# At most one kq and one kvt load under way in the retention, and two w1 loads

## The reference

```python
# q, k, v: 4 batches x 8 heads x 576 tokens x 64
scores = q @ k.T / sqrt(64)
ret = scores * D            # D[i, j] = gamma_head ** (i - j) for i >= j, else 0
x = (ret @ v)               # -> 2304 tokens x 512
h = x @ w_in                # 512 x 2048
g = where(h >= 1, h, where(h <= -1, 0, (h + 1) ** 2 / 4))
x = g @ w_out               # 2048 x 512
out = ((x @ w_a) * (x @ w_b)) @ w_out2    # 512 x 1536, 1536 x 512
```

## Time and profile before

| | |
|---|---|
| runs | 885.16, 887.18, 887.47 us |
| profiled execution | 886.08 us, of which the span 884.1 us |
| PE / PEld / DVE / ACT / POOL busy | 866.7 / 774.3 / 481.0 / 334.8 / 36.7 us |
| granted TensorE clock | 1.00 over the span |
| DMA | 137.46 MB, mean 155 GB/s |
| loads of the retention, us from issue to landing (median) | kq 6.7, kvt 5.9, w1 8.4 |

### The profile page before, as it was taken

How to read it: one execution, slowest core, us unless ns; L and a number is a source line. 1 busy time by engine, 2 the same in 40 slices (tenths; PEclk the granted TensorE clock), 3 DMA queues, 4 the chain that set the end, 5 groups by cost and what they waited for, 6 DMA issues and landing times.

```text
span 884.1 us, 13516 instructions
## 1 busy us (share of the span) xinstructions
PE 866.7 (98%) x5488; PEld 774.3 (88%) x5488; DVE 481.0 (54%) x831; ACT 334.8 (38%) x598; POOL 36.7 (4%) x54
## 2 busy tenths in 40 slices
PE   6889999999999999999999999999999999999998
PEld 6887888888899888888889999999999999999996
DVE  4685665655566755565663633574434574434443
ACT  1235555444454644444442433342223242223220
POOL 4550000000000000000000000000000000000000
PEclk9999999999999999999999999999999999999999
DMA  9997000023233022222345644545454845454622
GB/s 355 313 339 297 0 1 1 22 111 113 113 151 136 8 110 112 114 114 108 138 167 179 251 166 162 197 152 203 153 204 165 275 168 214 167 215 167 222 64 71
DMA packets 33453, 137.46 MB, mean 155 GB/s; under 512 B 2672, under 2 KB 12912, under 8 KB 28784
## 3 DMA queue, kind: packets, MB, share of 16 engines
q1 hardware_dynamic: 33248, 136.27, 42.2%
q10 hardware_dynamic: 144, 0.33, 0.1%
HBM read 109.86 MB, written 26.74 MB: 154 GB/s over the span
## 4 chain that ended last, share of the span: by engine, by line
PE 97%; DMA 1%; issue 1%; SPq 0%; DVE 0%; ACT 0%; POOL 0%; DVEq 0%; ACTq 0%; POOLq 0%
PE score_b L541 6%; PE score_b L545 6%; PE score_b L543 6%; PE score_a L545 4%; PE score_a L543 4%; PE score_a L541 4%; PE score_a L495 4%; PE kv_b L512 4%; PE score_b L495 4%; PE ret_b L512 4%; PE score_a L497 4%; PE score_a L496 4%; PE kv_b L513 4%; PE kv_b L514 4%; PE score_b L496 4%; PE ret_b L513 4%
## 5 line engine op out<-in xcount | busy, mean ns | idle before, releaser
L739 DVE TENSOR_TENSOR gate_w<-relu_s,relu_r 128x512 f32<-128x512 f32 (+1 forms) x80 | 51.0, 638 | 99.1 <-ACT relu_r L917 99.0
L541 PE MATMUL score_b<-xop_hi,wop 128*128 128x384 f32 x288 | 96.8, 336 | 0.1
L545 PE MATMUL score_b<-xop_hi,wop 128*128 128x384 f32 x288 | 96.7, 336 | 0.0
L543 PE MATMUL score_b<-xop_lo,wop 128*128 128x384 f32 x288 | 96.5, 335 | 0.0
L926 ACT ACTIVATE gh<-gated 128x512 fp32r<-128x512 f32 (+1 forms) x80 | 47.2, 590 | 105.9 <-DVE gated L742 105.9
L748 DVE TENSOR_TENSOR gl<-gated,gh 128x512 fp32r<-128x512 f32 (+1 forms) x80 | 51.1, 639 | 50.8 <-ACT gh L926 50.6
L541 PE MATMUL score_a<-xop_hi,wop 128*128 128x384 f32 x216 | 72.2, 334 | 0.0
L545 PE MATMUL score_a<-xop_hi,wop 128*128 128x384 f32 x216 | 72.2, 334 | 0.0
L543 PE MATMUL score_a<-xop_lo,wop 128*128 128x384 f32 x216 | 72.2, 334 | 0.0
L976 ACT ACTIVATE p<-score_b 128x384 f32<-128x384 f32 x36 | 17.7, 491 | 105.3 <-PE score_b L545 105.3
L541 PEld LDWEIGHTS score_b<-xop_hi,wop 128*128 128x128 f32 x288 | 54.1, 188 | 2.0 <-ACT p L976 0.4
(11 more groups left out here) (131 smaller groups left out, 2141.6 us busy)
## 6 DMA issues: line engine op xcount, KB each, us to landing
wop<-w_ops SPq DMA_DIRECT2D x36, 1792.0 KB, 7.3
w_ops<-op_hi SPq DMA_DIRECT2D x12, 896.0 KB, 4.6
w_ops<-op_lo SPq DMA_DIRECT2D x12, 896.0 KB, 6.4
kq<-k_q SPq DMA_DIRECT2D x16, 576.0 KB, 6.7
wo_raw<-w_out SPq DMA_DIRECT2D x9, 1024.0 KB, 9.7
kvt<-kv_tok SPq DMA_DIRECT2D x16, 512.0 KB, 5.9
ab_raw<-w_ab SPq DMA_DIRECT2D x12, 512.0 KB, 3.6
w1a_raw<-w SPq DMA_DIRECT2D x10, 512.0 KB, 8.4
```

The costliest lines, as they stand in the source:

```text
L541: pe.matmul(o, w[:, 0, at], xop_hi[b][:, k, :], start=(start and k == 0), stop=False, skip_group_check=True)
L543: pe.matmul(o, w[:, 0, at], xop_lo[b][:, k, :], start=False, stop=False, skip_group_check=True)
L545: mm = pe.matmul(o, w[:, 1, at], xop_hi[b][:, k, :], start=False, stop=(k == 1), skip_group_check=True)
L739: nc.vector.tensor_tensor(gate_w[:, 0:WIDTHS[t]], relu_s[:, 0:WIDTHS[t]], relu_r[:, 0:WIDTHS[t]], ALU.add).then_inc(gatew_ready, 1)
```

## The change

Three waits are added, all on SP. Before `kq` of unit n it waits until `kq` of unit n-1 has landed, before `kvt` of unit n until `kvt` of unit n-1 has landed, and before `w1` block f until block f-2 has landed. Nothing else is altered.

```diff
                     sp.wait_ge(scores_ready, 2 * (n - SLOTS) + 2)
                     sp.wait_ge(q_ready, n - SLOTS + 1)
+
+                if n:
+                    sp.wait_ge(kq_loaded[(n - 1) % SLOTS], 16 * ((n - 1) // SLOTS + 1))
                 sp.dma_start(kq[:, s, :, :], k_q[n]).then_inc(kq_loaded[s], 16)
                 if n >= SLOTS:
                     sp.wait_ge(kv_ready, n - SLOTS + 1)
                     sp.wait_ge(inner_done, n - SLOTS + 1)
+                if n:
+                    sp.wait_ge(kvt_loaded[(n - 1) % SLOTS], 16 * ((n - 1) // SLOTS + 1))
                 sp.dma_start(kvt[:, s, :, :, :], kv_tok[n]).then_inc(kvt_loaded[s], 16)
                 sp.dma_start(vtail[0:TAIL, s, :], v_tail[n]).then_inc(vtail_loaded[s], 16)
 
             def load_w1(f):
+                if f >= 2:
+                    sp.wait_ge(w1_loaded[f - 2], 16)
                 sp.dma_start(w1_raw(f), w1[f]).then_inc(w1_loaded[f], 16)
```

## The result

The changed kernel takes 901.34 us (median of 4 runs, 898.70 to 903.25), the kernel before 887.06: the ratio is 1.0163, with a 95% interval of 1.0133 to 1.0193. It is slower, by 1.3 to 1.9%, and outside the range that I gave. The profiled execution took 898.70 us, its span is 896.8 against 884.1 us.

What follows compares the result with a forecast made beforehand. PE bounds the kernel, with loads mattering only in the retention, the first 76 us; +0.5 us for a later hidden(0, 0) and +0.3 for a remaining stall gave +0.8, 888.0 us by the median, range 883.2 to 893.5.

Steps and rivals of the forecast that it cites:

- the period of a unit: Retention: each kq leaves only when its predecessor has landed, so a unit costs one full latency, 3.82 us (3.70 to 4.02).
- The third rival: Retention: serialised loads fall behind, as exposed latencies and code packets lie on the kq chain; +3.8 to +10.7 us, chance 0.28.
- Code packets: Retention: PE's instruction packets on queue q8 delay loads by 0 to 1.0 us each; 2.1 us taken on the kq chain.
- The end of the stage: Retention's end: w1 1 lands 1.4 us behind kvt 15, rounding, split and masks follow; hidden(0, 0) at 71.8 us, +0.5.
- w1 further on: After the retention: w1 loads two at a time, w1 9 near 83 us, last w1b near 95, cost 0.
- `load_ab`: After the retention: load_ab(0) comes some 5 us late, first used in the second token chunk, cost 0.
- The order of the first loads: Retention's start: nothing ahead of the first unit changes; decay masks leave at 8 and 12 us, mask 3 lands near 16.
- The signs: Expected in the trace: SP waiting on kq, POOL on kvt, DMA share near 0.8, ACT's wait near 3 us, later stretches unchanged.
- "PE falls back to its slow pace": Rival, retention: gaps bring back half-speed matmuls, a unit needs 5.9 us; +8 us if it lasts four units; chance 0.03.
- "The stalls go and the loads keep up": Rival, retention: 6.16 us of code stalls vanish, hidden(0, 0) at 65.2 us, 881 us by the median; chance 0.12.
- "The waits don't bind": Rival, retention: spread-out loads land in under 3.3 us, so nothing changes but the start; 0 us, chance 0.04.
- the two pages of the Trainium skill: Set against the rows: DMA time as 2.0 us plus bytes over 436 GB/s; crossing a code block "mostly hidden".

Runs made afterwards that it cites:

- e4: Kernel before, kvt waiting for its unit's kq and the next kq for that kvt, so one large load under way: 947.36 us against 886.48, ratio 1.0685.
- e1: The changed kernel without its w1 wait, keeping the kq and kvt waits: 902.98 us against 886.48 for the kernel before, ratio 1.0175.
- e2: The kernel before with the w1 wait alone: 884.23 us against 886.48, ratio 0.9988.
- e13: Kernel before, per unit a 1 KB load, then kq, kvt once the 1 KB has landed, next unit when all have landed: 934.55 us, one run.
- the seven kernels of the table: The kernel before, e3, e9, e11, e12, e14 and e15, whose loads keep up; the table sets their code stalls beside the start of hidden(0, 0).
- e7: Kernel before, kq and kvt of a unit issued together once both of the unit before have landed: 913.95 us against 887.16, ratio 1.0296.
- e3: The changed kernel with looser waits, each for the load before the last one (n-2, f-4): 885.43 us against 886.48 for the kernel before, ratio 0.9984.
- e9: Kernel before, at most three w1 loads under way up to block 9 and one for blocks 10 to 15: 885.02 us against 886.67, ratio 0.9982.
- e11: The looser waits of e3, with w1 1 and 2 moved behind units 13 and 14: 886.00 us against 886.67 for the kernel before, ratio 0.9986.
- e12: The kernel before with w1 1 and 2 moved behind units 13 and 14, no waits added: 886.86 us against 886.67, ratio 1.0003.
- e5: The kernel before with the wait ahead of kq alone: 897.00 us against 887.16, ratio 1.0113.
- e14: Kernel before with at most two kq, two kvt and three w1 loads under way: 884.72 us against 886.53, ratio 0.9974.
- e15: Kernel before with at most three w1 loads under way throughout, no kq or kvt waits: 884.83 us against 886.53, ratio 0.9989.

## Why the prediction was wrong

**The step that failed** is the period of a unit. I took 3.82 us, a load alone plus SP's reaction, with 4.02 as the upper end. Measured: `kq` 4.8 us median (3.6 to 5.1), 4.73 us a unit. From `kvt` 0 (6.67 us) to `kvt` 15 (78.66 us) it is 15x4.80 us where I had 15x3.96 with the code packets in it: 12.6 us more. `hidden(0, 0)` came 12.15 us behind the forecast 71.8, since `kvt` 0 had landed 0.4 us early; so this is the whole error. The latency alone was right (3.76 predicted, 3.7 measured in e4); what was wrong is the sentence that a second load half a period away does not touch it ("since one other load is behind each `kq`"). The nearest row was at hand and read the wrong way: a `kvt` in the retention itself, with a `kq` under way, took 4.5 us, and I used it only for when `kvt` 15 lands now.

**The third rival** was the right one in its sign and in most of its mechanism: latency, once exposed, isn't made up. I gave it 0.28. Its threshold (0.15 us a unit) held, its price did not: it had +3.8 us from latency alone and +10.7 at the most, and the median came out at +14.3.

**Code packets.** I priced them at 2.1 us on the chain. e4 leaves them little: from unit 4 on its `kq` takes 3.7 us at the median both in the six units with a code packet under way beside it and in the six without. Two `kvt` in whose first microsecond a packet started took 4.0 and 4.3 us and not 3.5. In the changed kernel nearly every load has a packet beside it, so nothing separates the two there. Their effect on PE did leave the chain, as foretold (the waits still list 1.6 us of it, in 2 pieces, for PEld), and that is worth nothing since PE waits for data.

**The end of the stage** came out: from `kvt` 15 to `hidden(0, 0)` 5.3 us predicted (66.5 to 71.8) and 5.3 measured (78.66 to 83.95), through `w1` 1, landed 1.5 us behind `kvt` 15 (1.4 predicted). In the chain it is the way over `copy_ret(13)` that stands, ending at 83.75, and 0.20 us later the masks release `hidden`; I had put half a microsecond between the two.

**w1 further on, `load_ab`, and all behind 84 us** cost 0, as forecast: e1 and e2 on either side, and the equal last stretch. They came far later than forecast (`w1` 9 at 99 us and not 83, the last at 112 and not 95, `load_ab(0)` issued 27 us later than before and not 5), so the cover held and the sums for it did not. The order of the first loads was as written, the masks came in time.

**The signs.** SP's long waits, POOL's wait in every unit and the equal stretches behind came as written. ACT's wait for `w1` 1 was 6.2 us and not 3. The DMA share from 16 to 64 us, foretold near 0.8, was 0.82, but that is luck: at 4.73 us a unit the engines move 254 GB/s, and the long packets at the beginning of each load (e13) are an estimated 0.17 of the share (0.4 us of engine time twice in 4.73).

**"PE falls back to its slow pace"**, 0.03 in my chances, did happen. In the changed kernel the granted clock is down for 3.4 us:

```profile
63.00:67.00 4.00, 1.74 (x61) 1.60 (x54) 1.70 (x5) 0.44 (x1) 2.09 (x3) 1.00 0.95 348
67.00:70.60 3.60, 3.60 (x60) 3.48 (x58) 0.84 (x3) 1.16 (x3) 1.55 (x3) 0.53 0.79 264
```

0.53 is the mean of 3.4 us at 1.2 and a little at 2.4 GHz. PE had been busy for 1.74 of the 4 us before. In this execution it cost nothing, since the chain went through the loads. In e1's it fell from 82.9 to 89.7, across the end of the stage and the first products of the layer:

```profile
82.90:89.70 6.80, 5.50 (x40) 5.00 (x41) 4.72 (x9) 3.25 (x6) 0.00 (x0) 0.50 1.02 415
```

There `hidden(0, 0)` came 7.5 us behind `kvt` 15 and not 5.3, 0.7 of which is `w1` 1 landing later. It falls at another place in the profiled execution of each kernel; the runs of the changed kernel with 898.70 and 903.25 us have mean clocks of 0.998 and 0.994. That is the likely source of the 1.7 us that the median (+14.3) has beyond the profiled execution (+12.6); no run here takes it away.

The reading on which that case rested was wrong, too. The record of the granted clock begins at 16.60 us in the kernel before, so the 1.00 beside the slow matmuls at 5.78 us says nothing of them; at 19.86 us the same 18 matmuls take 0.56 us. In the changed kernel the record begins at 19.3 us, and the 18 still take 1.00 us at 17.96 and 0.56 at 21.94. This cost nothing either, since the chain goes through the loads.

**"The stalls go and the loads keep up"** holds for looser limits only, and in part. "The waits don't bind" fell: every wait bound.

On the two pages of the Trainium skill that I had set against the rows: the measured 3.5 us for 512 KB alone, confirmed by e4, stays above the 3.2 us that the fit in DMA: Bandwidth & Descriptors, "Anatomy of one DMA — SWDGE (gpsimd) path", gives as an estimate; the fit is one for DMAs of the GpSimd path, and these loads are issued by SP. And that crossing a code block is "mostly hidden" (Runtime: NRT & Kernel Launch, "Instruction fetch mechanics") is not so for PE in this stage: 3.9 to 7.2 us of stalls in the seven kernels of the table.

**What stays open.** The traces hold the start and the end of each DMA packet. In the changed kernel the first packet of a `kq` moves 0.96 us after its issue (median of units 4 to 15), as in e4 (0.97), but its last one ends at 4.45 us and not at 3.39. So the load does not start late, it is drawn out. The long packets at the beginning of each load are a part of that, since each engine now carries those of both loads. With them it takes 1.85 us of engine time for a `kq` and 1.68 for a `kvt`, 3.5 of the 4.73 us of a unit. Why a load's first packets take long unless it follows another one at once, and why the engines still stand idle in between, no run here tells.

## What to carry to other kernels

Before a queue of loads is limited, take the latency of a load from a moment at which as many others are under way as the limit will leave, not from one that travels alone, and compare it with the period of the engine that it feeds; if it is longer, the limit is a serial chain, and its loss is the difference times the number of loads. Here 512 KB loads needed four under way to fill the engines; a limit at that depth was free, at half of it it cost 14 us. Look for what the limit could give back at all (here at most the 6 us of code stalls; the kernels with looser limits won 1 to 2 us), and measure two or three depths rather than one.

## What the runs showed of the hardware

Latency of large loads is not start plus transfer once they are staggered: 512 KB took 3.5, 4.3, 4.8 and 5.9 us with one, two, three and four under way, and the same two loads cost 1.4 us from landing to landing when issued together, and 2.2 when the second left 1.33 us later (4.8+1.33-3.9). A load that leaves alone or well behind another has some 17 long packets at its beginning (0.5 us against 0.16 to 0.18); one that leaves 0.42 us behind another has none at the median (e4, e7). PE's code stalls are 0.2 to 2.8 us each, and their sum does not follow the limits on the loads (before 6.2, e3 5.4, e9 3.9, e11 6.2, e12 7.2). The granted clock fell to 1.2 GHz for 3.4 or 6.8 us in most of the kernels in which PE waited in each unit (nine times in e4; not in e5), and twice in e2, in which it did not; ahead of the last microseconds it did not fall in the profiled executions of before, e3, e9, e11, e12, e14 and e15. PE's half-speed matmuls at the very start were there in all, beside a granted clock printed as 1.00; its record begins only at 15.3 to 23.7 us.
